# Attention probabilities leave PSUM in two pieces, bank 0 and banks 1 and 2 together, without GpSimd

## The chip, the cores and the metric

The kernel runs on one core of one Trainium2 chip. The metric is the device time of one execution in microseconds (us), as the median of several runs. An execution takes in an attention stage, a mixer with routing, and an expert stage. The change is in the attention stage alone.

The engines are named as in the profile: PE is TensorE (PEld its weight loads), DVE VectorE, ACT ScalarE, POOL GpSimd, SP SyncE.

## The reference, cut to what matters

```python
B, H, S, D = 4, 8, 1152, 64
q_pool = q.reshape(B, H, S // 2, 2, D).mean(axis=3)          # 576 rows per head
scores = (1 / np.sqrt(D)) * np.matmul(q_pool, k.transpose(0, 1, 3, 2))
scores = scores - np.max(scores, axis=-1, keepdims=True)
attn = np.exp(scores)
attn = attn / (np.sum(attn, axis=-1, keepdims=True) + 1e-09)
x = np.matmul(attn, v)                                       # 32 heads, then the mixer and the experts
```

All inputs are float32. Where the kernel multiplies on PE it splits an operand into a high part, rounded to `fp32r`, and a low part, the float32 value minus the high part, and adds up the products.

## The kernel before

The 32 heads are worked through as 16 pairs. A pair has 576 + 576 rows of queries, cut into nine row tiles n = 0 to 8 of 128 rows (tile 4 is shared by both heads). For every tile n of pair j, `tile = 9 * j + n`, and the engines do this:

- PE `score` (L466 to L475) makes the 128 x 1152 scores into three PSUM banks (`scores`). DVE `less_scores` (L615 to L620) reads them, writes `probs` and their row maximum. ACT `exp` (L567 to L572) turns `probs` into exponentials in place, two tiles ahead of their use.
- PE `turn` (L477 to L481) transposes the nine 128 x 128 blocks of `probs` into three PSUM banks, `ring[0]`, `ring[1]`, `ring[2]`, and counts `turned` up once per bank.
- The turned probabilities leave PSUM as `pt_h` (high) and `pt_l` (low). For banks 0 and 2 ACT writes `pt_h` with a copy of 384 columns (L592 to L596) and counts `high_done`; DVE writes `pt_l` by a subtraction (L682 to L686) and counts `low_done`. For bank 1 DVE copies the float32 values into an SBUF buffer `mid` (L679 to L681), and POOL makes both parts from there (`high` and `low`, L403 to L410).
- PE `weigh` (L483 to L499) multiplies `v_parts` with `pt_h` and `pt_l` for a group of two or three tiles, into the bank `acc`. ACT `acc_out` (L574 to L577) copies it to `out_t`; PE `fold` (L444 to L449) transposes that back into the bank `misc`; DVE `invert` (L625 to L633) and `fold_evac` (L635 to L652) divide by the row sums. `invert` begins with a small operation on 2 or 3 columns, L630.

Between these, PE transposes the k and q parts of the coming heads into the same bank `misc` (`prep`, L431 to L442), six pieces per head. A table `EXTRAS` (L176 to L186) gives every step n two slots, each with a `prep` or a `fold`. The first slot stands ahead of `score` on PE, and DVE empties `misc` after it; the second stands between `score` and `turn`, and ACT empties a `prep` of it. There is one bank `misc`, so a job waits until the one before it has been emptied (`extra_before`, L457).

The order on every engine is written out by hand. One step of it:

- PE (L520 to L539): job of slot 0; scores of tile n + 2, once DVE has read those of n + 1; job of slot 1; then, once DVE has counted `low_done` for the tile before, `turn` of tile n; then some of `weigh`.
- ACT (L584 to L598): `acc_out`, if one is due; evacuation of a `prep` in slot 1; the two copies of `pt_h`; `exp` of tile n + 2.
- DVE (L662 to L686): evacuation of slot 0, with `invert` ahead of it if it is a `fold`; `less_scores` of tile n + 2; the copy into `mid`; the two subtractions.
- POOL (L375 to L418): the work on `mid` of this tile, and between the tiles the splitting of k, q and v of the coming heads (`split_k`, `split_q`, `split_v`).

In every pair the steps 0, 3, 4, 5 and 7 have a `prep` in both slots; step 1 has fold 2 and then a `prep`; step 8 has fold 1 and then a `prep`; step 2 has fold 3 in slot 1 only, step 6 fold 0 in slot 0 only. The loops over the pairs repeat the same steps, so that the pairs in the middle of the stage look alike in the trace.

Of the kernel before, what the change touches and what calls it, by code (L numbers as in the profile page):

```python
# [7 lines left out]
F32 = mybir.dt.float32  # L8
# [88 lines left out]
def attention(nc, ctx, q, k, v, x_dram, shape_consts, consts, consts_loaded, w_in, stage, win_h):  # L97
# [8 lines left out]
    def sb(name, shape, dt=F32):  # L106
        return ctx.enter_context(nc.sbuf_tensor(name, shape, dt))
# [4 lines left out]
    def sem(name):  # L112
# [17 lines left out]
    q_t = [sb(f"q_t{i}", [P, 2, QT * P], F32R) for i in range(2)]  # L130

    probs = [sb(f"probs{i}", [P, NC, CK]) for i in range(3)]
    mid = [sb(f"mid{i}", [P, CK]) for i in range(3)]
# [12 lines left out]
    ring = [pb(f"ring{i}") for i in range(NC)]  # L146
    acc = pb("acc")
    misc = pb("misc")


    first_banks = [misc, acc, *ring]
    names = ("kA_loaded kB_loaded qA_loaded qB_loaded vA_loaded vB_loaded cleared pool_step split_done "
             "v_split mid_step mid_split pool_go prep_done prep_evac prep_evac_v scores_done neg_done exp_done turned "
             "win_loaded win_hi high_done low_done mid_done av_done acc_evac fold_done fold_evac sum_step x_stored")
# [97 lines left out]
    with nc.Block() as block:  # L252
# [65 lines left out]
        @block.gpsimd  # L318
        def _(pool):

            pool.sem_inc(s["mid_split"], 3)
# [8 lines left out]
            def split_k(par, head, j, part):  # L330

                if part == 0:
                    pool.wait_ge(k_loaded[par], 16 * (j + 1))
                    pool.sem_inc(s["pool_go"], 1)
                    high(k_parts[par][:, :, 0:DH], k_nat[par][:], s["pool_step"])
                else:
                    pool.wait_ge(s["pool_step"], 4 * head + 1)
                    low(k_parts[par][:, :, DH:2 * DH], k_nat[par][:], k_parts[par][:, :, 0:DH], s["pool_step"])

            def split_q(par, head, j, part):  # L340

                if part == 0:
                    pool.wait_ge(q_loaded[par], 32 * (j + 1))
                    nc.gpsimd.tensor_tensor(
                        q_sums[par][:], q_nat[par][:, :, 0], q_nat[par][:, :, 1], ALU.add
                    ).then_inc(s["pool_step"], 1)
                elif part == 1:
                    pool.wait_ge(s["pool_step"], 4 * head + 3)
                    pool.sem_inc(s["pool_go"], 1)
                    high(q_parts[par][:, :, 0:3:2], q_sums[par][:].unsqueeze(2).to_broadcast([P, QT, 2, DH]),  # L350
                         s["pool_step"])
                else:
                    pool.wait_ge(s["pool_step"], 4 * head + 4)
                    low(q_parts[par][:, :, 1], q_sums[par][:], q_parts[par][:, :, 0], s["split_done"])

            def split_v(par, head, j, part):
                if part == 0:
                    pool.wait_ge(v_loaded[par], 16 * (j + 1))
                    pool.sem_inc(s["pool_go"], 1)
                    high(v_parts[par][:, :, 0:DH], v_nat[par][:], s["mid_step"])  # L360
                else:
                    low(v_parts[par][:, :, DH:2 * DH], v_nat[par][:], v_parts[par][:, :, 0:DH], s["v_split"])


# [7 lines left out]
            pool.wait_ge(s["mid_step"], 1)  # L372
            split_v(0, 0, 0, 1)

            def step(j, n, after):  # L375
                tile = NT * j + n


                if n == 0 and after:
                    split_k(0, 2 * j + 2, j + 1, 0)  # L380
                    split_k(0, 2 * j + 2, j + 1, 1)
                elif n == 1 and after:
                    split_q(0, 2 * j + 2, j + 1, 0)
                    split_q(0, 2 * j + 2, j + 1, 1)
                elif n == 2 and after:
                    split_q(0, 2 * j + 2, j + 1, 2)
                elif n == 3:
                    if after:
                        split_k(1, 2 * j + 3, j + 1, 0)
                    split_v(1, 2 * j + 1, j, 0)  # L390
                elif n == 4:
                    split_v(1, 2 * j + 1, j, 1)
                    if after:
                        split_k(1, 2 * j + 3, j + 1, 1)
                elif n == 5 and after:
                    split_q(1, 2 * j + 3, j + 1, 0)
                    split_q(1, 2 * j + 3, j + 1, 1)
                elif n == 6 and after:
                    split_q(1, 2 * j + 3, j + 1, 2)
                elif n == 8 and after:  # L400
                    split_v(0, 2 * j + 2, j + 1, 0)

                highs = tile + 1 + 2 * j + (1 if n < 3 else 2) + (1 if n == 8 and after else 0)  # L403
                pool.wait_ge(s["mid_done"], tile + 1)
                pool.sem_inc(s["pool_go"], 1)
                cols = slice(n * P, (n + 1) * P)
                src = mid[n % 3][:].rearrange("p (i r) -> p i r", i=3)
                high(pt_h[:, 3:6, cols], src, s["mid_step"])
                pool.wait_ge(s["mid_step"], highs)
                low(pt_l[:, 3:6, cols], src, pt_h[:, 3:6, cols], s["mid_split"])  # L410
                if n == 8 and after:
                    split_v(0, 2 * j + 2, j + 1, 1)
                if n >= NT - KD and not after:

                    if n == NT - KD:
                        pool.wait_ge(s["win_loaded"], 16)
                    k = n - NT + KD
                    high(win_h[:, k], stage[:, k * DF:(k + 1) * DF], s["win_hi"])  # L418
# [11 lines left out]
        def _(pe):  # L430
# [45 lines left out]

            def turn(n, c):  # L477
                for i in range(3):
                    mm = nc.tensor.transpose(ring[c][:, i * P:(i + 1) * P],  # L479
                                             probs[n % 3][:, c, i * P:(i + 1) * P], ident)  # L480
                mm.then_inc(s["turned"], 1)  # L481

            def weigh(g, pair, turn):  # L483

                a, b, par, last, _ = GROUPS[g]
                if turn == 0:
                    pe.wait_ge(s["acc_evac"], 4 * pair + g + 1)
                    pe.wait_ge(s["v_split"], 2 * pair + par + 1)
                    pe.wait_ge(s["low_done"], 2 * (NT * pair + last + 1) + 2)
                for kt in range(*TURNS[g][turn:turn + 2]):  # L490
                    if kt == 3:

                        pe.wait_ge(s["mid_split"], NT * pair + last + 1 + 3)
                    for part in (pt_h, pt_l):
                        mm = nc.tensor.matmul(acc[:, 0:b - a], v_parts[par][:, kt], part[:, kt, a:b],  # L495
                                              start=(kt == 0 and part is pt_h),
                                              stop=(kt == KT - 1 and part is pt_l))
                if turn == len(TURNS[g]) - 2:
                    mm.then_inc(s["av_done"], 1)  # L499
# [52 lines left out]
        def _(act):  # L552
# [31 lines left out]
            def step(j, n, before, after):  # L584
# [4 lines left out]
                job = extra(j, n, 1, before, after)  # L589
                if job and job[0] == "prep":  # L590
                    prep_evac(job[1], job[2], job[3])
                for i, c in enumerate((0, 2)):  # L592
                    act.wait_ge(s["turned"], 3 * tile + c + 1)
                    nc.scalar.copy(pt_h[:, 3 * c:3 * c + 3, n * P:(n + 1) * P],  # L594
                                   ring[c][:, 0:CK].rearrange("p (i r) -> p i r", i=3)
                                   ).then_inc(s["high_done"], 1)  # L596
                if n + 2 < NT or after:
                    exp(tile + 2, (n + 2) % NT)  # L598

# [7 lines left out]
        def _(dve):  # L607
# [54 lines left out]
            def step(j, n, before, after):  # L662
# [13 lines left out]
                    less_scores(tile + 2, (n + 2) % NT)  # L676
                if folds[1] is not None:
                    fold_evac(folds[1], pair)
                dve.wait_ge(s["mid_split"], tile + 1)  # L679
                dve.wait_ge(s["turned"], 3 * tile + 2)  # L680
                nc.vector.tensor_copy(mid[n % 3][:], ring[1][:, 0:CK]).then_inc(s["mid_done"], 1)  # L681
                for i, c in enumerate((0, 2)):  # L682
                    dve.wait_ge(s["high_done"], 2 * tile + i + 1)
                    nc.vector.tensor_tensor(  # L684
                        pt_l[:, 3 * c:3 * c + 3, cols], ring[c][:, 0:CK].rearrange("p (i r) -> p i r", i=3),
                        pt_h[:, 3 * c:3 * c + 3, cols].bitcast(F32), ALU.subtract).then_inc(s["low_done"], 1)  # L686

            def tail(j):
                for g in (2, 3):
# [1101 lines left out]
```

## Time and profile before

| | |
|---|---|
| median of 3 runs | 1278.07 us (1275.68 to 1281.27) |
| span of the profiled execution | 1274.0 us |
| attention stage in it | from the start to about 590 us |
| busy share of the span: PE, PEld | 92%, 83% |
| busy share of the span: DVE, ACT, POOL | 62%, 45%, 42% |
| busiest lines of the attention stage | `less_scores` L618, `score` L472, `exp` L570 |

The span is the time from the first to the last instruction of one execution, taken by the profiler; the runs of the table's first row are timed without it. A duration in the profile is that of one instruction in this execution. "Idle before" is how long an engine stood still ahead of an instruction, and the name behind the arrow is the instruction that ended the wait. PE's own ends are modelled, so the gaps of its weight loads (PEld) show better when it waits.

### The profile page before, as it was taken

To read this page: it belongs to the slowest core of one execution; us is meant where nothing else is said; L and a number is where in the kernel's file an instruction comes from. 1 tells how busy PE (TensorE), PEld (TensorE's weight loads), DVE (VectorE), ACT (ScalarE), POOL (GpSimd) and SP (SyncE) were. 2 spreads that over 40 slices of the span, in tenths; PEclk is the share of its full clock that TensorE was granted. 3 is DMA by queue.
4 is the path that set the end of the run, shared out by engine and by line. 5 is a ranking of instruction groups with operands and counts; after the bars stand their busy time and mean duration, and the time that the engine had idled before them with its cause. 6 is when DMAs were issued, how large, how long until landed. Compare 5 with 4: busy or idle time off the path is not lost. (4 is left out here: it accounts for less than half of the span.)

```text
span 1274.0 us, 23890 instructions
## 1 busy us (share of the span) xinstructions
PE 1168.8 (92%) x7459; PEld 1051.3 (83%) x7460; DVE 785.7 (62%) x1501; ACT 567.0 (45%) x1022; POOL 535.4 (42%) x596
## 2 busy tenths in 40 slices
PE   6999999999999999997889999999718999799994
PEld 5999999999999999996778979888616788578783
DVE  4888888988888888896532634436235523443431
ACT  4666666666666666662412223222014411432320
POOL 6777777777777777753100010100013510440400
PEclk9999999999999999998899999999858999899997
DMA  5121221212111121102301020110057421531110
GB/s 188 44 65 56 65 65 47 65 56 65 39 63 62 59 65 61 31 9 75 95 1 38 1 75 0 55 64 6 32 162 264 172 83 40 207 107 37 34 41 21
DMA packets 49546, 86.39 MB, mean 68 GB/s; under 512 B 8110, under 2 KB 20526, under 8 KB 49520
## 3 DMA queue, kind: packets, MB, share of 16 engines
q1 hardware_dynamic: 39264, 52.49, 13.2%
q0 software_dynamic: 5952, 19.95, 4.6%
q10 hardware_dynamic: 4304, 13.64, 2.9%
q8 instruction: 13, 0.21, 0.1%
q14 instruction: 13, 0.11, 0.0%
HBM read 69.77 MB, written 17.33 MB: 68 GB/s over the span
## 5 line engine op out<-in xcount | busy, mean ns | idle before, releaser
L618 DVE TENSOR_SCALAR_CACHE_REDUCE probs<-scores 128x1152 f32<-128x1152 f32 x144 | 195.5, 1357 | 62.1 <-PE scores L472 61.1
L472 PE MATMUL scores<-k_t,q_t 128*128 128x384 f32 x960 | 202.0, 347 | 1.4 <-DVE probs L618 1.3
L570 ACT ACTIVATE probs<-probs,neg_max 128x1152 f32<-128x1152 f32 x144 | 181.8, 1262 | 0.0
L594 ACT CAST pt_h<-ring 128x384 fp32r<-128x384 f32 x288 | 138.9, 482 | 73.7 <-PE ring L479 67.9
L495 PE MATMUL acc<-pt_h,v_parts 128*128 128x256 f32 (+1 forms) x576 | 169.4, 316 | 0.6 <-DVE pt_l L684 0.6
L479 PE MATMUL ring<-consts,probs 128*128 128x128 f32 x1296 | 165.3, 273 | 0.7 <-DVE pt_l L684 0.7
L472 PEld LDWEIGHTS scores<-k_t,q_t 128*128 128x128 f32 x960 | 161.0, 189 | 2.2 <-DVE probs L618 2.1
L495 PE MATMUL acc<-pt_l,v_parts 128*128 128x256 f32 (+1 forms) x576 | 157.2, 295 | 0.0
L328 POOL TENSOR_TENSOR pt_l<-mid,pt_h 128x384 fp32r<-128x384 f32 x144 | 145.4, 1010 | 12.0
L479 PEld LDWEIGHTS ring<-consts,probs 128*128 128x128 f32 x1296 | 146.3, 141 | 2.4 <-DVE pt_l L684 1.8
L684 DVE TENSOR_TENSOR pt_l<-ring,pt_h 128x384 fp32r<-128x384 f32 x288 | 145.8, 548 | 0.0
L863 POOL DMA_INDIRECT sorted_tokens<-y,slot x20 | 19.2, 959 | 291.0 <-DVE y L1311 286.2
L325 POOL TENSOR_SCALAR pt_h<-mid 128x384 fp32r<-128x384 f32 x144 | 73.7, 512 | 133.6 <-DVE mid L681 131.8
L495 PEld LDWEIGHTS acc<-pt_h,v_parts 128*128 128x128 f32 x576 | 108.6, 189 | 0.9 <-ACT out_t L577 0.9
L495 PEld LDWEIGHTS acc<-pt_l,v_parts 128*128 128x128 f32 x576 | 109.0, 189 | 0.0
L1684 DVE TENSOR_TENSOR ht_l<-ht_ps,ht_h 128x512 fp32r<-128x512 f32 x44 | 30.4, 691 | 105.0 <-ACT ht_h L1614 105.0
L1508 POOL DMA_INDIRECT out<-result,index x22 | 23.3, 1058 | 159.1 <-DVE result L1739 157.7
L681 DVE COPY mid<-ring 128x384 f32<-128x384 f32 x144 | 79.6, 553 | 1.8 <-PE ring L479 1.8
L1553 PE MATMUL first_ps<-w_h,xt_h 128*128 128x512 f32 x176 | 71.6, 407 | 9.4 <-DVE w_l L1697 8.0
L1561 PE MATMUL second_ps<-w_h,ht_h 128*128 128x512 f32 x176 | 74.2, 422 | 6.3 <-DVE ht_l L1684 6.3
L1553 PE MATMUL first_ps<-w_l,xt_h 128*128 128x512 f32 x176 | 72.9, 414 | 0.0
L1475 POOL TENSOR_TENSOR w_l<-w_raw,w_h 128x1024 fp32r<-128x1024 f32 x20 | 51.6, 2608 | 47.2 <-ACT w_h L1630 47.1
(194 smaller groups left out, 2523.7 us busy)
## 6 DMA issues: line engine op xcount, KB each, us to landing
w_raw<-moe_w POOLq DMA_DIRECT2D x10, 1024.0 KB, 6.8
k_nat<-k SPq DMA_DIRECT2D x32, 288.0 KB, 2.8
v_nat<-v SPq DMA_DIRECT2D x32, 288.0 KB, 2.8
q_nat<-q SPq DMA_DIRECT2D x32, 256.0 KB, 2.9
w_raw<-moe_w ACTq DMA_DIRECT2D x3, 2048.0 KB, 10.2
rows_in<-sorted_tokens SPq DMA_DIRECT2D x23, 257.0 KB, 2.7
x_in<-x_heads SPq DMA_DIRECT2D x18, 256.0 KB, 3.3
x_heads<-x_pair SPq DMA_DIRECT2D x16, 256.0 KB, 2.3
```

The costliest lines, as they stand in the source:

```text
L325: nc.gpsimd.tensor_scalar(out, src, 1.0, 1.0, ALU.mult, ALU.mult).then_inc(signal, 1)
L328: nc.gpsimd.tensor_tensor(out, src, high_part.bitcast(F32), ALU.subtract).then_inc(signal, 1)
L472: mm = nc.tensor.matmul(scores[:, c, 0:CK], q_t[par][:, side, t * P:(t + 1) * P], k_t[par][:, c * CK:(c + 1) * CK], start=(i == 0), stop=( ...
L479: mm = nc.tensor.transpose(ring[c][:, i * P:(i + 1) * P], probs[n % 3][:, c, i * P:(i + 1) * P], ident)
L495: mm = nc.tensor.matmul(acc[:, 0:b - a], v_parts[par][:, kt], part[:, kt, a:b], start=(kt == 0 and part is pt_h), stop=(kt == KT - 1 and p ...
L570: nc.scalar.activation(probs[n % 3][:], probs[n % 3][:], ACT.Exp, bias=neg_max[:, n % 3:n % 3 + 1], scale=-1.0, accum_out=row_sum[:, n:n + ...
L594: nc.scalar.copy(pt_h[:, 3 * c:3 * c + 3, n * P:(n + 1) * P], ring[c][:, 0:CK].rearrange("p (i r) -> p i r", i=3)).then_inc(s["high_done"], 1)
L618: nc.vector.tensor_scalar(probs[n % 3][:], scores[:, :, 0:CK], -0.5 * DH ** -0.5, None, ALU.mult, ALU.min, accum_out=neg_max[:, n % 3:n % ...
L681: nc.vector.tensor_copy(mid[n % 3][:], ring[1][:, 0:CK]).then_inc(s["mid_done"], 1)
L684: nc.vector.tensor_tensor(pt_l[:, 3 * c:3 * c + 3, cols], ring[c][:, 0:CK].rearrange("p (i r) -> p i r", i=3), pt_h[:, 3 * c:3 * c + 3, co ...
L1553: mm = nc.tensor.matmul(first_ps[half][:], a[:, k], w[:, k, cols], start=(i == 0), stop=(i == 3 * KD - 1))
L1561: mm = nc.tensor.matmul(second_ps[:], a[:, k], w[:, k], start=(k == 0 and n == 0), stop=(k == K2 - 1 and n == 2))
```

## The change

`mid` goes, and with it POOL's work on the probabilities and its semaphores. `ring` becomes one PSUM tensor of three banks. A table `PARTS` names the two pieces in which it is emptied: bank 0, and banks 1 and 2 together. ACT copies both pieces into `pt_h` (384 and 768 columns), and DVE subtracts both into `pt_l`. The second copy waits for `turned` of bank 2, as the copy of bank 2 did. POOL, which was held to the pace of the tiles by `mid`, now only splits k, q and v; it gets waits of its own before it overwrites `k_parts` and `q_parts` (`prep_done`) and `v_parts` (`acc_evac`).

```diff
+    ring = ctx.enter_context(nc.psum_tensor("ring", [P, NC, 512], F32))
+    PARTS = ((0, 1), (1, NC))
...
@@ POOL: split_k, split_q, split_v
                 if part == 0:
                     pool.wait_ge(k_loaded[par], 16 * (j + 1))
+                    if head > 1 if isinstance(head, int) else True:
+                        pool.wait_ge(s["prep_done"], 12 * j - 9 + 6 * par)
...
                 if part == 0:
                     pool.wait_ge(v_loaded[par], 16 * (j + 1))
+                    if not (isinstance(j, int) and j == 0):
+                        pool.wait_ge(s["acc_evac"], 4 * j + 1 - 2 * (1 - par))
                     pool.sem_inc(s["pool_go"], 1)
...
-                high(pt_h[:, 3:6, cols], src, s["mid_step"])
-                pool.wait_ge(s["mid_step"], highs)
-                low(pt_l[:, 3:6, cols], src, pt_h[:, 3:6, cols], s["mid_split"])
...
@@ PE: weigh
-                    if kt == 3:
-
-                        pe.wait_ge(s["mid_split"], NT * pair + last + 1 + 3)
...
@@ ACT: step
-                for i, c in enumerate((0, 2)):
-                    act.wait_ge(s["turned"], 3 * tile + c + 1)
-                    nc.scalar.copy(pt_h[:, 3 * c:3 * c + 3, n * P:(n + 1) * P],
-                                   ring[c][:, 0:CK].rearrange("p (i r) -> p i r", i=3)
-                                   ).then_inc(s["high_done"], 1)
+                for a, b in PARTS:
+                    act.wait_ge(s["turned"], 3 * tile + b)
+                    nc.scalar.copy(
+                        pt_h[:, 3 * a:3 * b, n * P:(n + 1) * P].rearrange("p (c i) r -> p c i r", i=3),
+                        ring[:, a:b, 0:CK].rearrange("p c (i r) -> p c i r", i=3)).then_inc(s["high_done"], 1)
...
@@ DVE: step
-                dve.wait_ge(s["mid_split"], tile + 1)
-                dve.wait_ge(s["turned"], 3 * tile + 2)
-                nc.vector.tensor_copy(mid[n % 3][:], ring[1][:, 0:CK]).then_inc(s["mid_done"], 1)
-                for i, c in enumerate((0, 2)):
+                for i, (a, b) in enumerate(PARTS):
                     dve.wait_ge(s["high_done"], 2 * tile + i + 1)
                     nc.vector.tensor_tensor(
-                        pt_l[:, 3 * c:3 * c + 3, cols], ring[c][:, 0:CK].rearrange("p (i r) -> p i r", i=3),
-                        pt_h[:, 3 * c:3 * c + 3, cols].bitcast(F32), ALU.subtract).then_inc(s["low_done"], 1)
+                        pt_l[:, 3 * a:3 * b, cols].rearrange("p (c i) r -> p c i r", i=3),
+                        ring[:, a:b, 0:CK].rearrange("p c (i r) -> p c i r", i=3),
+                        pt_h[:, 3 * a:3 * b, cols].bitcast(F32).rearrange("p (c i) r -> p c i r", i=3),
+                        ALU.subtract).then_inc(s["low_done"], 1)
```

On DVE, step 3 in the loop before: evacuation of a `prep`, `less_scores`, the copy to `mid`, two subtractions, and the evacuation that opens step 4.

```order
L657 CAST k_t<-misc 128x384
L617 REGISTER_ALU
L618 TENSOR_SCALAR probs,neg_max<-scores 128x1152
L679 REGISTER_ALU
L680 ISA
L681 COPY mid<-ring 128x384
L683 ISA
L684 TENSOR_TENSOR pt_l<-ring,pt_h 128x3x128
L683 REGISTER_ALU
L684 TENSOR_TENSOR pt_l<-ring,pt_h 128x3x128
L655 REGISTER_ALU
L660 CAST q_t<-misc 128x512
```

The same place on DVE after (line numbers of the changed kernel):

```order
L647 CAST k_t<-misc 128x384
L607 REGISTER_ALU
L608 TENSOR_SCALAR probs,neg_max<-scores 128x1152
L670 ISA
L671 TENSOR_TENSOR pt_l<-ring,pt_h 128x3x128
L670 REGISTER_ALU
L671 TENSOR_TENSOR pt_l<-ring,pt_h 128x6x128
L645 REGISTER_ALU
L650 CAST q_t<-misc 128x512
```

Three operations of 384 columns have become one of 384 and one of 768, and each of the two now stands behind a copy of ACT.

On ACT, a step with a k piece in slot 1, before:

```order
L557 REGISTER_ALU
L559 CAST k_t<-misc 128x384
L593 ISA
L594 CAST pt_h<-ring 128x3x128
L593 REGISTER_ALU
L594 CAST pt_h<-ring 128x3x128
L569 REGISTER_ALU
L570 ACTIVATE probs,row_sum<-probs,neg_max 128x1152
```

and after:

```order
L547 REGISTER_ALU
L549 CAST k_t<-misc 128x384
L583 ISA
L584 CAST pt_h<-ring 128x3x128
L583 REGISTER_ALU
L584 CAST pt_h<-ring 128x6x128
L559 REGISTER_ALU
L560 ACTIVATE probs,row_sum<-probs,neg_max 128x1152
```

The second copy is twice as wide; `exp` stands behind it as before.

On POOL, the end of a pair and its loop before, with the semaphores that rows wait for. The v split of step 8 is cut in two by the work on `mid`:

```order
L325 TENSOR_SCALAR v_parts<-v_nat 128x9x64 [waits a_vA_loaded]
L404 REGISTER_ALU
L325 TENSOR_SCALAR pt_h<-mid 128x3x128 [waits a_mid_done]
L409 ISA
L328 TENSOR_TENSOR pt_l<-mid,pt_h 128x3x128 [waits a_mid_step]
L328 TENSOR_TENSOR v_parts<-v_nat,v_parts 128x9x64
L422 REGISTER_ALU
L422 COMPARE_AND_BRANCH
```

and after; the loop begins again with the k split of the next head, that is with a `TENSOR_SCALAR` and a `TENSOR_TENSOR` of `k_parts`:

```order
L325 TENSOR_TENSOR q_parts<-q_sum,q_parts 128x5x64 [waits a_pool_step]
L361 ISA [waits a_vA_loaded]
L322 TENSOR_SCALAR v_parts<-v_nat 128x9x64 [waits a_acc_evac]
L325 TENSOR_TENSOR v_parts<-v_nat,v_parts 128x9x64 [waits a_v_step]
L415 REGISTER_ALU
L415 COMPARE_AND_BRANCH
```

What holds this v split is now `acc_out` of group 1, which ACT does at the head of step 7; behind it v, k and q run without a wait for a tile.

## Rows read from the trace of the kernel before

**Rows 1.** Page, parts 1 and 2: busy us and share of each engine; granted clock in tenths.

```profile
PE 1168.8 (92%) x7459; PEld 1051.3 (83%) x7460; DVE 785.7 (62%) x1501; ACT 567.0 (45%) x1022; POOL 535.4 (42%) x596
...
PEclk9999999999999999998899999999858999899997
```

**Rows 2.** Busy time by stretch, four pairs of heads: stretch, length, busy of each engine, clock.

```profile
203.75:346.30 142.55, 142.08 (x1078) 137.75 (x1077) 126.55 (x254) 95.36 (x189) 105.96 (x129) 1.00 0.18 58
```

**Rows 3.** Waits of PE's weight loads, 60 to 560 us: us in total, times, longest.

```profile
PEld misc L441 <- DVE x_pair L649: 6.1, 15, 0.6
PEld misc L441 <- DVE k_t L657: 5.1, 14, 0.4
PEld misc L441 <- DVE q_t L660: 1.8, 12, 0.2
```

**Rows 4.** Timeline of steps 2 and 3: start, us, instruction, [idle before <- releaser].

```profile
207.57 0.48 ACT L594 CAST pt_h<-ring 128x384 fp32r<-128x384 f32 x1 [0.17 <-PE ring L479]
...
207.68 0.55 DVE L681 COPY mid<-ring 128x384 f32<-128x384 f32 x1
...
208.14 1.01 DVE L684 TENSOR_TENSOR pt_l<-ring,pt_h 128x384 fp32r<-128x384 f32 x2
...
208.31 1.00 PEld L472 LDWEIGHTS scores<-k_t,q_t 128*128 128x128 f32 x6
...
209.07 0.55 DVE L657 CAST k_t<-misc 128x384 fp32r<-128x384 f32 x1
...
209.67 0.31 PEld L441 LDWEIGHTS misc<-consts,k_parts 128*128 128x128 f32 x3 [0.36 <-DVE k_t L657]
```

**Rows 5.** Timeline of steps 3 to 5.

```profile
210.63 1.09 ACT L594 CAST pt_h<-ring 128x384 fp32r<-128x384 f32 x2
...
212.96 0.53 PEld L441 LDWEIGHTS misc<-consts,q_parts 128*128 128x128 f32 x4
...
214.25 0.98 ACT L594 CAST pt_h<-ring 128x384 fp32r<-128x384 f32 x2
...
216.01 0.68 DVE L660 CAST q_t<-misc 128x512 fp32r<-128x512 f32 x1
...
216.75 0.20 PEld L441 LDWEIGHTS misc<-consts,q_parts 128*128 128x128 f32 x2 [0.15 <-DVE q_t L660]
```

**Rows 6.** The one other ACT row that reads PSUM across two banks (whole trace, by line).

```profile
L1116 ACT ACTIVATE u_t<-wide 128x576 f32<-128x576 f32 x16 | 10.3, 649 | 26.3 <-PE wide L892 26.3
```

**Rows 7.** Timeline of steps 7 and 8.

```profile
223.83 0.40 ACT L577 COPY out_t<-acc 128x320 f32<-128x320 f32 x1
...
225.41 1.09 ACT L594 CAST pt_h<-ring 128x384 fp32r<-128x384 f32 x2
...
227.32 1.00 POOL L328 TENSOR_TENSOR pt_l<-mid,pt_h 128x384 fp32r<-128x384 f32 x1
...
227.38 0.97 DVE L630 TENSOR_SCALAR row_eps<-row_sum 128x2 f32<-128x2 f32 x1
...
229.02 0.31 PEld L441 LDWEIGHTS misc<-consts,k_parts 128*128 128x128 f32 x3 [0.39 <-DVE x_pair L649]
```

**Rows 8.** Timeline, POOL alone, at the end of a pair and the start of the next.

```profile
232.59 1.42 POOL L328 TENSOR_TENSOR v_parts<-v_nat,v_parts 128x576 fp32r<-128x576 f32 x1
233.97 0.68 POOL L325 TENSOR_SCALAR k_parts<-k_nat 128x576 fp32r<-128x576 f32 x1
234.73 1.44 POOL L328 TENSOR_TENSOR k_parts<-k_nat,k_parts 128x576 fp32r<-128x576 f32 x1
```

**Rows 9.** Timeline of step 1 of the next pair.

```profile
234.16 0.98 ACT L594 CAST pt_h<-ring 128x384 fp32r<-128x384 f32 x2
...
235.92 0.27 DVE L630 TENSOR_SCALAR row_eps<-row_sum 128x3 f32<-128x3 f32 x1
...
236.73 0.28 DVE L649 TENSOR_TENSOR x_pair<-misc,row_inv 128x128 f32<-128x128 f32 x1
...
237.21 0.32 PEld L441 LDWEIGHTS misc<-consts,q_parts 128*128 128x128 f32 x2
```

More of the change, by code:

```diff
@@ L132, in attention @@
     probs = [sb(f"probs{i}", [P, NC, CK]) for i in range(3)]
-    mid = [sb(f"mid{i}", [P, CK]) for i in range(3)]
     pt_h = sb("pt_h", [P, KT, NT * P], F32R)
@@ L145, in attention @@
     scores = ctx.enter_context(nc.psum_tensor("scores", [P, NC, 512], F32))
-    ring = [pb(f"ring{i}") for i in range(NC)]
+    ring = ctx.enter_context(nc.psum_tensor("ring", [P, NC, 512], F32))
     acc = pb("acc")
     misc = pb("misc")
-    first_banks = [misc, acc, *ring]
+    first_banks = [misc, acc, *(ring[:, c] for c in range(NC))]
     names = ("kA_loaded kB_loaded qA_loaded qB_loaded vA_loaded vB_loaded cleared pool_step split_done "
-             "v_split mid_step mid_split pool_go prep_done prep_evac prep_evac_v scores_done neg_done exp_done turned "
-             "win_loaded win_hi high_done low_done mid_done av_done acc_evac fold_done fold_evac sum_step x_stored")
+             "v_split v_step pool_go prep_done prep_evac prep_evac_v scores_done neg_done exp_done turned "
+             "win_loaded win_hi high_done low_done av_done acc_evac fold_done fold_evac sum_step x_stored")
     s = {n: sem("a_" + n) for n in names.split()}
@@ L319, in _ @@
         def _(pool):
-            pool.sem_inc(s["mid_split"], 3)
             def high(out, src, signal):
@@ L347, in split_q @@
                 elif part == 1:
+                    if head > 1 if isinstance(head, int) else True:
+                        pool.wait_ge(s["prep_done"], 12 * j - 6 + 6 * par)
                     pool.wait_ge(s["pool_step"], 4 * head + 3)
@@ L358, in split_v @@
                     pool.wait_ge(v_loaded[par], 16 * (j + 1))
+                    if not (isinstance(j, int) and j == 0):
+                        pool.wait_ge(s["acc_evac"], 4 * j + 1 - 2 * (1 - par))
                     pool.sem_inc(s["pool_go"], 1)
-                    high(v_parts[par][:, :, 0:DH], v_nat[par][:], s["mid_step"])
+                    high(v_parts[par][:, :, 0:DH], v_nat[par][:], s["v_step"])
                 else:
+                    pool.wait_ge(s["v_step"], head + 1)
                     low(v_parts[par][:, :, DH:2 * DH], v_nat[par][:], v_parts[par][:, :, 0:DH], s["v_split"])
@@ L371, in _ @@
             split_v(0, 0, 0, 0)
-            pool.wait_ge(s["mid_step"], 1)
             split_v(0, 0, 0, 1)
             def step(j, n, after):
-                tile = NT * j + n
                 if n == 0 and after:
@@ L401, in step @@
                     split_v(0, 2 * j + 2, j + 1, 0)
[L403 to L407, printed above, removed]
-                high(pt_h[:, 3:6, cols], src, s["mid_step"])
-                pool.wait_ge(s["mid_step"], highs)
-                low(pt_l[:, 3:6, cols], src, pt_h[:, 3:6, cols], s["mid_split"])
                 if n == 8 and after:
@@ L478, in turn @@
                 for i in range(3):
-                    mm = nc.tensor.transpose(ring[c][:, i * P:(i + 1) * P],
+                    mm = nc.tensor.transpose(ring[:, c, i * P:(i + 1) * P],
                                              probs[n % 3][:, c, i * P:(i + 1) * P], ident)
```

## The prediction

> **What bounds the kernel now.** I read the page first, then the busy time by stretch, then the waits of PE, then the timeline of one pair of heads. On the page PE is busy for 92% of the span and its clock stands at the upper of its two levels (2.4 GHz) over the whole attention stage [rows 1]. In a stretch of four pairs PE is busy 142.08 of 142.55 us, with the clock at 1.00; DVE follows with 126.55, then POOL with 105.96 and ACT with 95.36 [rows 2]. So the attention stage is PE's, and an engine that is relieved gives nothing back by itself. PE's true idleness is what its weight loads show: 6.1 + 5.1 + 1.8 = 13.0 us in 500 us, all of it on the bank `misc`, which DVE has not yet emptied [rows 3]. About once in every pair each of these waits occurs (15, 14 and 12 times in 14 pairs). That is the first bound: if all of PE's waits went, 16 pairs would give back 16 x 13.0 / 14 = 15 us and no more.
>
> The waits come about in this way [rows 4]. DVE's two subtractions of step 2 end at 208.14 + 1.01 = 209.15; the k piece of step 3's first slot, which PE had put into `misc`, is copied from 209.07 to 209.62; PE's scores were all issued at 208.31 + 1.00 = 209.31, and its second `prep` starts at 209.67, 0.36 late. **So what counts is when DVE's last subtraction of a tile ends**, in those steps that have a job of DVE in slot 0 and a `prep` in slot 1: 3, 4, 5, 7, 8, 0 and 1.
>
> **What is removed.** DVE's copy to `mid` (0.47 us from its start to the next operation's, 207.68 to about 208.14) and POOL's two operations per tile. DVE's subtractions were 0.47 and 0.55 us [rows 4]. From 384 to 512 columns a DVE evacuation grows from 0.55 to 0.68 [rows 4, 5], about 1 ns per column, so that one of 768 takes an estimated 0.95. DVE's work per tile thus goes from 0.47 + 0.47 + 0.55 = 1.49 to 0.47 + 0.95 = 1.42: 0.07 saved, almost nothing.
>
> **What is added to the path.** ACT's second copy grows from 384 to 768 columns, and DVE's last subtraction has to wait for all of it. Before, DVE worked on the copy to `mid` and on bank 0 meanwhile, and ACT's second copy was over before DVE asked for it. The price of the copy: 0.48 for 384 columns [rows 4], 0.649 for 576 in the only row that reads PSUM over two banks [rows 6]; the slope is 0.88 ns per column and gives 0.649 + 0.17 = 0.82 for 768. The bounds are 0.65 (the 576 columns themselves) and 0.96 (two copies of 0.48 end to end); I take 0.82, since the nearer row is that of 576. From ACT's end to DVE's start I take 0.04, as from DVE's end to PE's (209.62 to 209.67).
>
> Step 3, written out [rows 4]: the last bank is ready for ACT at 207.57; copy until 208.39; DVE's wide subtraction 208.43 to 209.38 (DVE itself would be ready at 207.68 + 0.47 = 208.15, so it is ACT that decides); the k copy begins 0.08 before that end, as now, at 209.30, and ends at 209.85; PE starts at 209.90. Now it starts at 209.67: **0.23 later**.
>
> Step 4 [rows 5]: ACT's two copies end at 210.63 + 1.09 = 211.72, so the second began at 211.24. After: copy to 212.06, subtraction 212.10 to 213.05, k copy 212.97 to 213.52, PE at 213.57 instead of 212.96, where it did not wait at all: **0.61 later**. Step 5: second copy from 214.25 + 0.98 - 0.48 = 214.75 to 215.57, subtraction to 216.56, the q copy (0.68) from 216.48 to 217.16, PE at 217.22 instead of 216.75: **0.47 later**.
>
> Step 1 [rows 9]: second copy from 234.66 to 235.48, subtraction to 236.47, then the chain of the fold. From the end of its first operation (235.92 + 0.27 = 236.19) to the end of `x_pair` (237.01) it takes 0.82; begun at 236.39 and with 0.2 for the first operation, it ends at 237.41, and PE starts at 237.46 instead of 237.21: **0.25 later**. Steps 7 and 0, read in the same way, come out at nothing and at about 0.1: their weighing before the scores is longer or the piece itself arrives late. I take **0.1** for both.
>
> **The term that can go either way** is step 8 [rows 7]. There DVE's small operation L630 on two columns takes 0.97 us, from 227.38 to 228.35, and POOL's subtraction runs from 227.32 to 228.32. In rows 9 the same line takes 0.27 and ends at 236.19, when POOL's subtraction of rows 8 ends (234.73 + 1.44 = 236.17). So L630 doesn't get through while a POOL operation that began before it is running. PE waits 0.39 at 229.02 behind that. The Trainium skill, page "SBUF — State Buffer", section "Who interferes with whom", says that VectorE and GpSimd share a pair of ports as an exclusive lock, which the one that starts first keeps for its whole instruction, and names tensor_scalar among the operations that take it. By that rule the dropping of POOL's work would count for the change, and the trace agrees with the lock; it leaves open what POOL does at that moment afterwards.
>
> If POOL is idle then: ACT's second copy of step 7 from 225.41 + 1.09 - 0.48 = 226.02 to 226.84, subtraction to 227.83, L630 from 227.75 to 227.95, and PE could start 0.67 later (as from 228.35 to 229.02), at 228.62, when its scores are just issued (229.02 - 0.39 = 228.63). The wait is gone: **0.39 earlier**.
>
> But POOL, freed of the tiles, now runs v, then k, then q in one go, and starts when `acc_out` of step 7 is done. That copy ends now at 224.23 [rows 7], and stands behind ACT's longer copy, so at 224.57. With 0.1 for the semaphore, v's first half starts at 224.67; from a first half to its second 0.76, from a second half to the next first half 1.38 [rows 8]. So k's second half starts at 224.67 + 0.76 + 1.38 + 0.76 = 227.57 and runs 1.44, to 229.01, and L630 asks at 227.75: **inside it**, 0.18 after its start. L630 ends at about 229.04, PE starts at 229.71: **0.69 later**. No tile's pace holds POOL any more, so this falls out alike in every pair, or in none. With 0 to 0.2 for the semaphore k's second half starts between 227.47 and 227.67, still before 227.75; a longer ACT copy moves both sides alike.
>
> **The sum.** Per pair 0.23 + 0.61 + 0.47 + 0.25 + 0.1 = 1.66, and 0.69 from step 8: 2.35 us. The last pair has no `prep` from step 3 on, so 15 pairs count: 35 us. The first tiles and the last pair, in which `turn` itself waits for the subtraction, I estimate at 1 us more, a few times 0.1 to 0.4. Split operations of POOL, its new waits and the loads behind them cost nothing: k and q are split most of a pair ahead of their `prep`. What hides them is that lead; were it gone, PE would wait at step 3 or 7. `exp` ends 0.34 later and has a whole tile of slack. The clock stays at its upper level: waits of 0.6 us in a tile of 4 us are of the kind PE already has. The profiled execution had a span of 1274.0, the median is 1278.07, 4 us more. So 1274 + 35 + 1 + 4 = **1314 us**.
>
> **The rivals.**
> *POOL misses L630.* For it: only 0.18 us lie between. If POOL's extra wait instructions cost 0.2 more, or DVE's wide subtraction is that much shorter, the hold is gone. Then 1.66 - 0.39 = 1.27 per pair, 19 us: 1274 + 19 + 1 + 4 = 1298.
> *The wide copy costs hardly more than the narrow one* (the side on which it is not slower). If ACT's copy over two banks takes 0.48, DVE's own order decides in steps 3, 7 and 0; the terms become about -0.05, 0.27, 0.13, -0.07 and, with POOL also missed, -0.39: -0.1 per pair, 1276. It decides from about 0.5 us down. Against it speaks the row of 576 columns at 0.649.
> *The work saved on DVE comes through.* If DVE's total set the pace, 0.07 x 144 tiles = 10 us would be gained: 1268; with all of PE's waits gone the limit is 1278 - 15 = 1263. Against it: DVE is busy 126.55 of 142.55 us. The Trainium skill, page "VectorE: DVE Perf Modes", section on the TRN2 errata, advises operations of 512 columns or more, since a fixed cost is paid per operation; it speaks for this change. The rows show that fixed cost as the 0.07 per tile above.
> *A dearer copy.* At 0.96 six terms grow by 0.14: 13 us, 1327.
>
> **How the numbers follow.** L630 held 48%, POOL misses it 37%, no change 7%, gain 3%, dearer or another wait 5%. A measurement of this kernel tells 0.5% (6 us) from no change: faster 0.03, same 0.07, slower 0.90. The range reaches from the second case less some 8 us for a copy of 0.73 to the first case with a copy 0.09 dearer: 1290 to 1322. The likeliest case alone: 1306 to 1322.
>
> **What would show it.** PE's waits on DVE `k_t` and `q_t` of about 0.6 at steps 3, 4 and 5; ACT's wide copy at 0.82 and DVE's at 0.95, with DVE waiting on ACT before the latter; L630 at step 8 at over 1 us beside POOL's `k_parts`; the stage's end some 35 us later. It would be wrong if the copy takes 0.5, if POOL is elsewhere, or if PE waits on POOL.

## The result, and the profile after

The changed kernel takes 1308.34 us (median of 4 runs, 1304.84 to 1309.19), the kernel before beside it 1278.62: a ratio of 1.0232 with an interval of 1.0211 to 1.0253, so 29.7 us slower. The forecast was 1314, with 1290 to 1322 as its range.

The page of the changed kernel, its parts 1, 2 and 5 (line numbers here and below are those of the kernel that is shown; L671 is the subtraction, L684 before, and L584 ACT's copy, L594 before):

```profile
span 1307.5 us, 22899 instructions
...
PE 1179.3 (90%) x7459; PEld 1050.4 (80%) x7460; DVE 776.2 (59%) x1357; ACT 612.4 (47%) x1022; POOL 323.0 (25%) x308
...
PEclk9999999999999999999789999999857999899998
...
L671 DVE TENSOR_TENSOR pt_l<-ring,pt_h 128x384 fp32r<-128x384 f32 (+1 forms) x288 | 217.5, 757 | 58.8 <-ACT pt_h L584 55.5
```

Beside [rows 1]: POOL's work fell from 535 to 323 us, DVE's by 10 and ACT's rose by 45; PE's weight loads took the same time, 1050.4 and 1051.3, in a span that is 33.5 us longer. The clock stood at its upper level throughout the attention stage, as before. DVE now waits 55.5 us for ACT's copy.

The store of `x_heads` by SP marks the pairs, after and then before:

```profile
217.69 0.37 SPq L271 DMA_DIRECT2D x_heads<-x_pair  x1
255.29 0.37 SPq L271 DMA_DIRECT2D x_heads<-x_pair  x1
```

```profile
208.41 0.37 SPq L272 DMA_DIRECT2D x_heads<-x_pair  x1
244.04 0.37 SPq L272 DMA_DIRECT2D x_heads<-x_pair  x1
```

A pair took 35.63 us and takes 37.60, and the same for every pair in the middle of the stage: 1.97 more. The last group of weight loads of the stage starts at 617.30 instead of 588.43, 28.9 later. The other 4.6 us by which the profiled spans differ lie behind the stage, where the code is the same; the medians, 29.7 apart, don't show them, so I take them for the scatter of one execution.

PE's waits, 60 to 560 us, in total, times and longest, and what [rows 3] showed of before:

```profile
PEld misc L434 <- DVE x_pair L639: 16.9, 27, 1.1
PEld misc L434 <- DVE k_t L647: 15.4, 27, 0.6
PEld misc L434 <- DVE q_t L650: 7.8, 13, 0.6
```

40.1 us instead of 13.0. All are waits for the bank `misc`: those of before at steps 3, 5 and 8 have grown, and steps 4 and 1, where PE hardly waited or not at all, have one in every pair. No weight load waits for POOL.

### The profile page after: what moved, and what is told of

The parts are those of the page before. It is cut to its first block and busy times, and to the rows that moved or that the text cites. A ratio compares the mean times of both kernels' runs of the same rounds, so it can differ in the third digit from the quotient of the medians.

```text
span 1307.5 us, 22899 instructions
## 1 busy us (share of the span) xinstructions
PE 1179.3 (90%) x7459; PEld 1050.4 (80%) x7460; DVE 776.2 (59%) x1357; ACT 612.4 (47%) x1022; POOL 323.0 (25%) x308
## 5 line engine op out<-in xcount | busy, mean ns | idle before, releaser
L671 DVE TENSOR_TENSOR pt_l<-ring,pt_h 128x384 fp32r<-128x384 f32 (+1 forms) x288 | 217.5, 757 | 58.8 <-ACT pt_h L584 55.5
L584 ACT CAST pt_h<-ring 128x384 fp32r<-128x384 f32 (+1 forms) x288 | 185.0, 642 | 62.9 <-PE ring L472 56.7
L322 POOL TENSOR_SCALAR v_parts<-v_nat 128x576 fp32r<-128x576 f32 x32 | 21.5, 672 | 365.0 <-ACT out_t L567 365.0
L1542 PE MATMUL first_ps<-w_h,xt_l 128*128 128x512 f32 x176 | 70.9, 403 | 0.0
L1550 PE MATMUL second_ps<-w_l,ht_h 128*128 128x512 f32 x176 | 69.6, 395 | 0.0
L1550 PE MATMUL second_ps<-w_h,ht_l 128*128 128x512 f32 x176 | 69.5, 395 | 0.0
L434 PE MATMUL misc<-consts,k_parts 128*128 128x128 f32 x273 | 47.0, 281 | 23.6 <-DVE x_pair L639 10.9
```

The lines of the kernel that those rows point to most:

```text
L434: mm = nc.tensor.transpose(bank[:, i * P:(i + 1) * P], src.bitcast(F32), ident)
L584: nc.scalar.copy(pt_h[:, 3 * a:3 * b, n * P:(n + 1) * P].rearrange("p (c i) r -> p c i r", i=3), ring[:, a:b, 0:CK].rearrange("p c (i r) - ...
L671: nc.vector.tensor_tensor(pt_l[:, 3 * a:3 * b, cols].rearrange("p (c i) r -> p c i r", i=3), ring[:, a:b, 0:CK].rearrange("p c (i r) -> p ...
L1542: mm = nc.tensor.matmul(first_ps[half][:], a[:, k], w[:, k, cols], start=(i == 0), stop=(i == 3 * KD - 1))
L1550: mm = nc.tensor.matmul(second_ps[:], a[:, k], w[:, k], start=(k == 0 and n == 0), stop=(k == K2 - 1 and n == 2))
```

## Where the time of a pair went

Steps 2 to 5 of one pair after, timeline; they answer to [rows 4, 5]:

```profile
217.33 0.80 ACT L584 CAST pt_h<-ring 128x768 fp32r<-128x768 f32 x1 [0.17 <-PE ring L472]
...
218.16 0.96 DVE L671 TENSOR_TENSOR pt_l<-ring,pt_h 128x768 fp32r<-128x768 f32 x1 [0.18 <-ACT pt_h L584]
...
219.04 0.55 DVE L647 CAST k_t<-misc 128x384 fp32r<-128x384 f32 x1
...
219.64 0.31 PEld L434 LDWEIGHTS misc<-consts,k_parts 128*128 128x128 f32 x3 [0.57 <-DVE k_t L647]
...
223.52 0.42 PEld L434 LDWEIGHTS misc<-consts,q_parts 128*128 128x128 f32 x4 [0.57 <-DVE k_t L647]
...
227.64 0.20 PEld L434 LDWEIGHTS misc<-consts,q_parts 128*128 128x128 f32 x2 [0.60 <-DVE q_t L650]
```

The chain is the one that the prediction wrote out: ACT's wide copy takes 0.80, DVE's wide subtraction starts 0.03 behind its end, the k copy 0.08 before the end of the subtraction, and PE 0.05 behind the k copy. PE waits 0.57, 0.57 and 0.60 where it waited 0.36, nothing and 0.15.

Steps 7 and 8 after, timeline, in place of [rows 7]:

```profile
234.99 0.41 ACT L567 COPY out_t<-acc 128x320 f32<-128x320 f32 x1
...
235.59 0.67 POOL L322 TENSOR_SCALAR v_parts<-v_nat 128x576 fp32r<-128x576 f32 x1 [13.92 <-ACT out_t L567]
...
238.50 1.43 POOL L325 TENSOR_TENSOR k_parts<-k_nat,k_parts 128x576 fp32r<-128x576 f32 x1
...
238.63 1.33 DVE L620 TENSOR_SCALAR row_eps<-row_sum 128x2 f32<-128x2 f32 x1
...
240.62 0.31 PEld L434 LDWEIGHTS misc<-consts,k_parts 128*128 128x128 f32 x3 [1.10 <-DVE x_pair L639]
```

Step 1 of the same stretch, in place of [rows 9]:

```profile
248.02 0.16 DVE L620 TENSOR_SCALAR row_eps<-row_sum 128x3 f32<-128x3 f32 x1
...
249.05 0.20 PEld L434 LDWEIGHTS misc<-consts,q_parts 128*128 128x128 f32 x2 [0.19 <-DVE x_pair L639]
```

At steps 7 and 8 POOL waits 13.92 us for `acc_out` and then runs v and k in one go. DVE asks for L620, two columns, 0.13 us after the k subtraction has begun, and gets it 1.33 us later, at 239.96, when POOL's subtraction ends (239.93). PE waits 1.10.

From the first weight load of the scores to that of `turn`, step by step, before and after. Steps 2 and 6 did not change, and the sum of the differences is the whole of the longer pair:

| step | before | after | more | forecast |
|---|---|---|---|---|
| 3 | 1.64 | 1.85 | 0.21 | 0.23 |
| 4 | 1.48 | 1.96 | 0.48 | 0.61 |
| 5 | 1.33 | 1.77 | 0.44 | 0.47 |
| 7 and 0 | 2.87 | 2.92 | 0.05 | 0.1 |
| 8 | 1.67 | 2.37 | 0.70 | 0.69 |
| 1 | 1.28 | 1.36 | 0.08 | 0.25 |
| sum | | | 1.96 | 2.35 |

## The experiments

Two theories were on the table, as parts of one sum: the **joined piece** (a copy of 0.80 and a subtraction of 0.96 in a row behind the last bank), and the **hold** (POOL's k split holds L620 at step 8). The rivals: that it is POOL's lost help as such, that it is ACT's total work, or that the hold lies beside the path. All times are medians. The kernel before took 1279.85 us beside pool_later, early_invert, three_pieces and three_early, 1277.69 beside narrow_copies, extra_ahead, extra_behind and before_early, and 1280.15 beside last_single and before_early_again. So runs of different groups are compared by their ratios and, better still, by the length of a pair, which is the same to a few hundredths of a us in every pair in the middle of a trace.

| run | us | ratio to before (95%) | one pair, us |
|---|---|---|---|
| kernel before | 1278.62 | | 35.63 |
| changed kernel | 1308.34 | 1.0232 (1.0211 to 1.0253) | 37.60 |
| pool_later | 1292.82 | 1.0110 (1.0085 to 1.0134) | 36.6 |
| early_invert | 1293.86 | 1.0112 (1.0091 to 1.0134) | 36.53 |
| three_pieces | 1274.80 | 0.9969 (0.9953 to 0.9986) | 35.57 |
| three_early | 1276.29 | 0.9972 (0.9958 to 0.9986) | 35.57 |
| narrow_copies | 1282.69 | 1.0042 (1.0025 to 1.0059) | 36.03 |
| extra_ahead | 1306.67 | 1.0236 (1.0206 to 1.0265) | 37.49 |
| extra_behind | 1295.38 | 1.0147 (1.0118 to 1.0176) | 36.80 |
| last_single | 1304.34 | 1.0185 (1.0165 to 1.0205) | 37.2 |
| before_early | 1274.35 | 0.9977 (0.9956 to 0.9997) | 35.33 |
| before_early_again | 1275.82 | 0.9965 (0.9951 to 0.9980) | 35.3 |

**The hold, taken away on POOL's side.** POOL waits ahead of its k split:

```diff
                 if n == 8 and after:
                     split_v(0, 2 * j + 2, j + 1, 1)
+                    pool.wait_ge(s["fold_evac"], 4 * j + 2)
```

> The changed kernel, and POOL waits at the end of each pair until DVE has emptied fold 1, so that its k split can't lie beside L620 of step 8. Theory (two causes: ACT's wide copy ahead of DVE's wide subtraction, about 1.26 us per pair at the start of turn, and POOL's k split that holds L620, the rest): L620 back from 1.33 to about 0.16 us, PE's wait of 1.10 at step 8 gone, turn 0.9 us earlier there, 14 pairs x 0.9 = 13 us, 1308 to 1295. Rival (the hold is beside the path, or it isn't POOL that holds L620): 1308 as the changed kernel.

Measured 1292.82, 15.5 less than the changed kernel. DVE's code is unchanged; L621 is its L620:

```profile
233.16 0.16 DVE L621 TENSOR_SCALAR row_eps<-row_sum 128x2 f32<-128x2 f32 x1
```

```profile
234.72 0.68 POOL L322 TENSOR_SCALAR k_parts<-k_nat 128x576 fp32r<-128x576 f32 x1 [2.41 <-PE misc L435]
```

0.16 instead of 1.33, and the k split now begins behind it. PE has no wait at step 8, and those of steps 3, 4 and 5 stay at 0.57, 0.57 and 0.59. A pair is 1.0 us shorter, in 14 pairs 14 us. So it is POOL's operation that held L620, and the hold lay on the path. That the k split may wait here shows besides that POOL is far ahead.

**The hold, taken out of the chain on DVE's side.**

```diff
                 for g in folds:
-                    if g is not None:
+                    if g in (0, 3):
                         invert(g, pair)
                 if folds[0] is not None:
                     fold_evac(folds[0], pair)
+                    if folds[0] < 2:
+                        invert(folds[0] + 1, pair)
...
```

(and behind the last pair, where the `invert` of fold 2 goes, since step 8 has done it)

> The changed kernel, and DVE does the invert of fold 1 in step 6 and that of fold 2 in step 8, each behind the fold_evac that stands there, so that no invert lies between DVE's last subtraction and the emptying of misc. Theory: the wait at step 8 (1.10) goes whether or not POOL runs then, and that of step 1 (0.19): 14 x (0.92 + 0.08) = 14 us, 1308 to 1294, while the waits of steps 3, 4 and 5 stay at 0.57, 0.57 and 0.60. Rival (the waits move to the next step of DVE): no more than 5 us gained.

Measured 1293.86. PE's waits left in a pair:

```profile
214.10 0.31 PEld L434 LDWEIGHTS misc<-consts,k_parts 128*128 128x128 f32 x3 [0.57 <-DVE k_t L647]
...
217.97 0.42 PEld L434 LDWEIGHTS misc<-consts,q_parts 128*128 128x128 f32 x4 [0.57 <-DVE k_t L647]
...
222.09 0.20 PEld L434 LDWEIGHTS misc<-consts,q_parts 128*128 128x128 f32 x2 [0.59 <-DVE q_t L650]
```

L620 is still held, now at step 8 for fold 2 and for 0.96 us, but nobody waits for it there. A pair is 1.07 shorter than in the changed kernel: 0.99 at step 8, and 0.08 at step 1, where L620 was not held but stood in the chain. This is also the base on which the joining can be studied without the hold.

**POOL dropped, but nothing joined.**

```diff
-    PARTS = ((0, 1), (1, NC))
+    PARTS = ((0, 1), (1, 2), (2, NC))
...
-                    dve.wait_ge(s["high_done"], 2 * tile + i + 1)
+                    dve.wait_ge(s["high_done"], 3 * tile + i + 1)
```

(and PE's waits on `low_done` with 3 in place of 2 per tile)

> The changed kernel with PARTS of one bank each: ACT makes three copies of 384 columns and DVE three subtractions; POOL has no share, but nothing is joined. Theory (the joining costs, not the loss of POOL): waits at steps 3, 4, 5 back to those of the kernel before (0.36, 0, 0.15), 15 x 1.26 = 19 us less than the changed kernel, 1289; L620 at step 8 is asked for some 0.06 us beside the start of POOL's k split, so 1284 to 1289 if it is held and 1276 if not. Rival (POOL's help was needed, DVE or ACT is too full without it): 1300 or more.

Measured 1274.80: below the changed kernel by 33.5 us, and below the kernel before. The rival, that the kernel is slower because POOL's help was needed, is out. L620 was not held, and how near it came is to be seen in the timeline:

```profile
226.67 0.15 DVE L620 TENSOR_SCALAR row_eps<-row_sum 128x2 f32<-128x2 f32 x1
226.68 1.42 POOL L325 TENSOR_TENSOR k_parts<-k_nat,k_parts 128x576 fp32r<-128x576 f32 x1
```

L620 came 0.01 us ahead of POOL's subtraction here, 0.01 to 0.03 in all 14 pairs, and took 0.15 to 0.16. PE's waits at steps 4 and 5, though, are not those of before, which the expectation had them be:

```profile
208.72 0.31 PEld L434 LDWEIGHTS misc<-consts,k_parts 128*128 128x128 f32 x3 [0.36 <-DVE k_t L647]
...
209.69 1.25 ACT L584 CAST pt_h<-ring 128x384 fp32r<-128x384 f32 x3
...
210.21 1.49 DVE L671 TENSOR_TENSOR pt_l<-ring,pt_h 128x384 fp32r<-128x384 f32 x3
...
212.21 0.42 PEld L434 LDWEIGHTS misc<-consts,q_parts 128*128 128x128 f32 x4 [0.18 <-DVE k_t L647]
...
216.04 0.20 PEld L434 LDWEIGHTS misc<-consts,q_parts 128*128 128x128 f32 x2 [0.30 <-DVE q_t L650]
```

0.18 and 0.30 instead of nothing and 0.15 at steps 4 and 5: where ACT empties a `prep` first, its first copy ends only at 210.17, and DVE, which used to begin with a copy that needs nothing from ACT, waits for it.

**Both edits.** The pieces of `three_pieces` with the `invert` of `early_invert`.

> Both edits: pieces of one bank each, and invert of folds 1 and 2 early. Theory: waits as in the kernel before at steps 3, 4, 5, and none at step 8, where the kernel before has 0.39: 14 x 0.22 to 0.39 = 3 to 5 us under the kernel before, about 1274. Rival (POOL's share was worth its place): at or above the kernel before, 1279 or more.

Measured 1276.29, with a pair of 35.57 as in `three_pieces`; the difference of 1.5 us between the two is within their spread. The waits of 0.18 and 0.30 are there as well, against the expectation. With L620 off the path in both, moving it brought nothing more.

**Which half of the joined piece costs.** On the base of `early_invert`, ACT copies the banks singly and DVE still subtracts two together:

```diff
-                for a, b in PARTS:
+                for a, b in ((0, 1), (1, 2), (2, NC)):
...
-                    dve.wait_ge(s["high_done"], 2 * tile + i + 1)
+                    dve.wait_ge(s["high_done"], 3 * tile + b)
```

> As early_invert, but ACT copies banks 1 and 2 singly, while DVE still subtracts both in one operation of 768 columns behind the third copy. Theory (what costs is the length of the copy that stands behind the last bank, 0.80 instead of 0.48): DVE's wide subtraction starts 0.32 earlier, waits at steps 3, 4 and 5 of about 0.3, 0.25 and 0.3: 0.8 us per pair, 12 us less than early_invert, about 1282. Rival (the wide subtraction of DVE is the cost): as early_invert, 1294.

Measured 1282.69, which meets the forecast time, but in part by luck: the forecast was 0.8 us per pair and a pair became 0.50 shorter, 7.5 us in 15 pairs. By the ratios `early_invert` is 9 us away; the 11 between the two medians hold a kernel before that ran 2 us faster beside this run. The waits:

```profile
211.33 0.31 PEld L434 LDWEIGHTS misc<-consts,k_parts 128*128 128x128 f32 x3 [0.36 <-DVE k_t L647]
...
215.05 0.42 PEld L434 LDWEIGHTS misc<-consts,q_parts 128*128 128x128 f32 x4 [0.42 <-DVE k_t L647]
...
219.12 0.20 PEld L434 LDWEIGHTS misc<-consts,q_parts 128*128 128x128 f32 x2 [0.55 <-DVE q_t L650]
```

Only step 3 came about as forecast (0.36 for 0.3). Where ACT empties a `prep` ahead of its copies, three copies in a row take 1.25. That ends only 0.16 sooner than one narrow and one wide behind a k piece (1.41, which counts at step 4), and 0.05 sooner behind a q piece (1.30, which counts at step 5). The rest of the way to `three_early` (0.46 of 0.96 us per pair) is DVE's wide subtraction, which can't begin on bank 1 while bank 2 is still being copied. So both halves cost, about alike, 0.50 and 0.46; the rival, that the wide subtraction is the cost, was half right.

**Path or load.** On the base of `early_invert`, one more copy of 384 columns on ACT, constants into a scratch buffer: in `extra_ahead` ahead of the wide copy (shown), in `extra_behind` the same line behind both copies and ahead of `exp`:

```diff
                 for a, b in PARTS:
+                    if a:
+                        nc.scalar.copy(scratch[n % 3][:], consts[:, 0:CK])
                     act.wait_ge(s["turned"], 3 * tile + b)
```

> As early_invert, with one more ACT copy of 384 columns (constants into a scratch buffer) between the two copies of a tile, so ahead of the wide one. Theory: it fills the 0.17 us in which ACT waits for the last bank and delays the wide copy by some 0.2 to 0.3 in each of steps 3, 4, 5, 0, 1: 1.0 to 1.5 us per pair, 15 to 22 us over early_invert, about 1312. Rival (ACT has slack: 47% busy): no change, 1294.

> As extra_ahead, but the extra copy stands behind the wide one and ahead of exp: the same work on ACT off the path of the subtraction. Theory: exp ends 0.4 later and nobody waits: 1294 as early_invert, within 3 us. Rival (it is ACT's total work that counts, not its place): the same time as extra_ahead.

Measured 1306.67 and 1295.38. By the pair, that is 0.96 and 0.27 us over `early_invert`, 14 and 4 us in 15 pairs. (The medians are 12.8 and 1.5 apart, but the kernel before was 2 us faster beside these two; by the ratios it is 16 and 4.) The same work costs three to four times as much in the one place as in the other. From steps 3 and 4 with the copy ahead:

```profile
220.74 0.53 ACT L585 COPY scratch<-consts 128x384 f32<-128x384 f32 x1
...
221.15 0.81 ACT L587 CAST pt_h<-ring 128x768 fp32r<-128x768 f32 x1
...
222.00 0.96 DVE L676 TENSOR_TENSOR pt_l<-ring,pt_h 128x768 fp32r<-128x768 f32 x1 [0.56 <-ACT pt_h L587]
...
223.47 0.42 PEld L435 LDWEIGHTS misc<-consts,q_parts 128*128 128x128 f32 x4 [0.76 <-DVE k_t L650]
```

The forecast of 1.0 to 1.5 us per pair was a little too high. For `extra_behind` no loss was forecast, within 3 us. What it does lose, 0.27 per pair, is not at steps 3 to 5, where its waits are 0.58, 0.58 and 0.60, but here:

```profile
235.11 1.39 DVE L622 TENSOR_SCALAR row_eps<-row_sum 128x3 f32<-128x3 f32 x1
```

```profile
240.00 0.42 PEld L435 LDWEIGHTS misc<-consts,q_parts 128*128 128x128 f32 x4 [0.39 <-DVE q_t L652]
```

ACT is later, so POOL is later, and holds the moved `invert` of step 8 for 1.39 instead of 0.96; `less_scores` behind it comes late, and step 0 pays 0.39. A later `acc_out` moves the hold, even where the added work itself is free.

**The other cut.** `PARTS = ((0, 2), (2, NC))` on the base of `early_invert`: the wide piece first, the narrow one last.

> As early_invert, but the pieces are banks 0 and 1 together and bank 2 alone. Theory (what counts is when DVE's last subtraction ends, and here that is DVE's wide subtraction of 0.96, which starts behind ACT's wide copy, and then 0.55): ACT's wide copy can start only with bank 1, some 0.3 before the last bank, so DVE ends at about copy start + 0.80 + 0.04 + 0.88 + 0.55, 0.1 to 0.2 later than in early_invert: 1294 to 1297. Rival (only the work behind the last bank counts, and that is now a narrow copy): waits as in narrow_copies, 1283 or less.

Measured 1304.34, 10.5 over `early_invert`, and 0.67 per pair. The rival is out, but the time was missed, 1294 to 1297 being the forecast.

```profile
219.18 1.18 ACT L584 CAST pt_h<-ring 128x768 fp32r<-128x768 f32 x2 [0.17 <-PE ring L472]
...
220.01 1.42 DVE L673 TENSOR_TENSOR pt_l<-ring,pt_h 128x768 fp32r<-128x768 f32 x2 [0.86 <-ACT pt_h L584]
...
221.95 0.42 PEld L434 LDWEIGHTS misc<-consts,q_parts 128*128 128x128 f32 x4 [0.71 <-DVE k_t L647]
```

DVE starts 0.83 behind ACT's first copy and ends 1.42 later, 0.14 later than with the other cut: the waits are 0.70, 0.71 and 0.73 instead of 0.57, 0.57 and 0.59. So the delay of a step, 0.1 to 0.2, was forecast rightly, and the sum over the stage was not: three steps of 0.14 in 15 pairs are 6 us already. Left out altogether was that steps 7 and 0 lose as much (waits of 0.26 and 0.27); five steps of 0.14 in 15 pairs are the 10 us.

**The hold in the kernel before.** The edit of `early_invert` in the kernel before, with POOL's share and `mid` left as they were.

> The kernel before, with the invert of folds 1 and 2 moved as in early_invert, nothing else. Theory: the wait of 0.39 at step 8 goes, 3 to 5 us, 1274; waits of steps 3 and 5 stay. Rival (POOL's subtractions hold L630 at the new place and delay less_scores instead): 1279 as before.

> The kernel before_early once more, in more rounds, since its first interval (0.9956 to 0.9997) nearly touches no change. Theory: 0.31 us per pair, 5 us, ratio 0.996. Rival: no difference, ratio 0.999 or more.

Measured 0.9977 and 0.9965 of the kernel before, 0.31 us less per pair. The 0.39 at step 8 [rows 7] is gone, and what is left is what was to stay:

```profile
242.85 0.31 PEld L441 LDWEIGHTS misc<-consts,k_parts 128*128 128x128 f32 x3 [0.36 <-DVE k_t L657]
...
249.93 0.20 PEld L441 LDWEIGHTS misc<-consts,q_parts 128*128 128x128 f32 x2 [0.15 <-DVE q_t L660]
```

The rival, that the `invert` is held at its new place, came in part: that of fold 1 takes 0.47 there and that of fold 2 0.27 in its first operation, and no wait of PE comes of it. This is the shortest pair of all, 35.33; in time it can't be told from `three_pieces`.

**The account.** With L620 off the chain on both sides the pairs can be compared: 35.33 with POOL's share, 35.57 without it in single pieces, 36.53 joined. So of the 1.97 us by which the changed kernel's pair is longer, **0.96 is the joining, 0.24 the loss of POOL's share** (where ACT empties a `prep` first, DVE's first operation now waits for ACT), and the rest, 0.76 to 0.77, the `invert` in the chain: it costs 1.07 in the changed kernel and cost 0.31 before. Of this rest 0.70 is the longer hold at step 8, as in the table, and 0.08 is step 1. The split between joining and POOL's share holds for this order of work, in single edits; what either costs where the other isn't there was not measured.

## Why the prediction was right, step by step

- **PE sets the pace, and its waits for `misc` are what changes.** Right: the differences at the steps with these waits add up to the longer pair, 1.96 of 1.97, and PE waits for nothing else.
- **The wide copy at 0.82, the wide subtraction at 0.95.** Measured 0.80 and 0.96. The row of 576 columns over two banks [rows 6] was a good base; the bounds of 0.65 and 0.96 were wider than needed.
- **Steps 3, 4 and 5.** The waits came out at 0.57, 0.57 and 0.60, against 0.59, 0.59 and 0.62 in the working. But the cost was taken from the start of the second `prep`, and `turn` behind it is what counts. In step 4 the four transposes of the `prep` took 0.53 before [rows 5] and take 0.42 behind a wait, so that 0.1 of the wait is made good. The term was 0.61 and is 0.48.
- **Step 1** was mis-sized the most, 0.25 for 0.08. PE does wait there, 0.19 instead of 0.25; the first operation of `invert` takes 0.16 where no POOL operation stands beside it, and a part is made good as in step 4.
- **Step 8: held or not.** The case with 48% came. POOL's k split began 0.13 before L620 was asked for, against 0.18 in the working, and PE's `turn` is 0.70 later for 0.69. The semaphore from ACT to POOL took 0.19 (235.40 to 235.59), not the 0.1 that was taken; at some 0.32 the rival would have come. That it was a near thing is shown by `three_pieces`, which escaped by 0.01 to 0.03 us. The mechanism was right, but which of the two cases would come the working could not tell at a margin of 0.13 us, and 14 pairs of 1.0 us hang on it: that the time lies so near 1314 is in part luck.
- **The sum.** 2.35 per pair was 1.96: this, times 15, is the 6 us between 1314 and 1308. The hold occurs in 14 pairs, not 15: in the last round of POOL's loop L620 takes 0.16 at step 8, since no k split follows. That would be 0.7 us less, and the 1 us for the first tiles and the last pair is not to be found in the trace either: 15 pairs of 1.97 less 0.7 are the 28.9 by which the stage ends later.
- **The rivals.** "POOL misses L630" is what `pool_later` shows: a pair of 36.6, 0.97 over before where the working had 1.27, and 1292.82 where it had 1298. "The wide copy costs hardly more" and "a dearer copy" are out by the 0.80. "The work saved on DVE comes through" is out: DVE is busy 10 us less and the kernel is slower. The Trainium skill (page "VectorE: DVE Perf Modes", section on the TRN2 errata) advises operations of 512 elements or more, because each one pays a fixed cost. The page says this of operations that read SBUF, a condition that the prediction left out: DVE's subtraction reads `pt_h` there, but ACT's copy reads PSUM alone. The second piece met the advice, and three narrow pieces were faster by 0.96 us per pair. A fixed cost is there, 1.49 us for three subtractions in a row against 1.42 for a narrow and a wide one, but here the end of the last operation counts, not the sum.
- **The lock.** The Trainium skill (page "SBUF — State Buffer", section "Who interferes with whom") has whichever of the two engines comes first shut the other out. For POOL first the traces agree where it was 0.03 us ahead or more: L620 ended 0.02 to 0.03 us behind POOL's operation. For DVE first, as in `three_pieces`, they show only that L620 isn't held. That POOL is then shut out isn't to be seen: its subtraction took 1.41 to 1.43 there, as elsewhere. And at 0.01 us the recorded order decides nothing, as this place in the last pair of the kernel before shows, where L630 came second and wasn't held:

```profile
581.23 1.02 POOL L328 TENSOR_TENSOR pt_l<-mid,pt_h 128x384 fp32r<-128x384 f32 x1
581.24 0.16 DVE L630 TENSOR_SCALAR row_eps<-row_sum 128x2 f32<-128x2 f32 x1
```

## What to carry to other kernels

Where one engine's operation can begin only when another's has ended, a joined operation puts its whole length on the path. Small pieces let the two engines overlap, and the fixed cost that joining saves on an engine which isn't the bottleneck (here 0.07 us per tile on DVE) doesn't come back as time. An engine that is relieved of paced work may run its remaining work in a burst, as POOL did here, and the question is what stands beside that burst. A tiny operation that the burst can hold belongs where its engine waits anyway, not between two steps of the critical chain. And a near miss of 0.01 us, as in `three_pieces`, is a reason to move such an operation even where it costs nothing yet.

## What the runs showed of the hardware

- A DVE operation on two or three columns of SBUF took 0.16 us alone and up to 1.39 us when a POOL subtraction had begun 0.04 us or more before it; it ended 0.02 to 0.03 us behind POOL's. DVE's subtractions and copies out of PSUM kept their length beside POOL (0.55, 0.96).
- ACT's copy out of PSUM took 0.48 us for 384 columns and 0.80 for 768; three of 384 in a row took 1.25, so that each further one costs 0.38.
- From the end of ACT's or DVE's operation to the start of the one that waits for it: 0.03 to 0.05 us on DVE and PE, 0.19 on POOL.
